# Attention, spatial gating and a feed-forward on one core: weights by output halves, VectorE turns of the late weights, four token staging tiles

## The reference, cut to what matters

```python
# attention: B=2, H=8, S=768, D=64; 8 global keys, 96 local keys, linear bias per head
scores = q @ k.T / 8 + bias; keep = is_global | is_local
x = softmax(where(keep, scores, -1e9)) @ v             # -> [2, 768, 512]
h = relu(x @ w_in)                                     # 512 -> 1024
u, v = h[..., :512], h[..., 512:]
v_n = (v - mean(v)) / sqrt(var(v) + 1e-6)              # over the 512 columns
x = (u * (w_spatial @ v_n + b_spatial[:, None])) @ w_out   # w_spatial 768 x 768
u = x + (x.T @ U @ V).T                                # rank 32 over the sequence
out = u + relu(u @ w_ch1) @ w_ch2                      # 512 -> 2048 -> 512
```

## Time and profile before

| | us |
|---|---|
| median of 3 runs | 559.49 |
| the three runs | 559.15, 559.49, 563.11 |
| profiled execution | 562.82 |
| its span | 560.7 |
| PE busy | 533.7 (95%) |
| VectorE busy | 289.5 (52%) |
| ScalarE busy | 174.3 (31%) |
| GpSimd busy | 112.0 (20%) |
| mean granted clock of TensorE | 0.98 of full speed |

### The profile page before, as it was taken

One profiled execution on the slowest core, in us unless ns is written; L12 is line 12 of the kernel. 1 busy time (PEld: TensorE's weight loads), 2 busy tenths in 40 slices (PEclk: granted clock), 3 DMA queues, 4 the chain that ended last, 5 costly groups with the idle time before them and its releaser, 6 DMA issues.

```text
span 560.7 us, 7652 instructions
## 1 busy us (share of the span) xinstructions
PE 533.7 (95%) x2728; PEld 418.3 (75%) x2728; DVE 289.5 (52%) x845; ACT 174.3 (31%) x429; POOL 112.0 (20%) x134
## 2 busy tenths in 40 slices
PE   7688999899999999999989999999999999999996
PEld 5455666567777788878768888888888888888884
DVE  5748888857775534689822265523146524011012
ACT  4755665645555533332311101021010102101010
POOL 5884000000000001498389500000000000000000
PEclk8969999989999999999989999999999999999999
DMA  7975454545514000055223100002000002000002
GB/s 179 226 158 130 102 102 105 119 97 130 122 47 129 29 30 0 2 168 161 84 76 112 39 0 1 0 1 75 1 0 2 0 2 75 1 0 1 0 1 79
DMA packets 45835, 36.25 MB, mean 65 GB/s; under 512 B 29504, under 2 KB 39744, under 8 KB 45792
## 3 DMA queue, kind: packets, MB, share of 16 engines
q1 hardware_dynamic: 39776, 19.34, 15.6%
q0 software_dynamic: 3216, 11.63, 6.9%
q10 hardware_dynamic: 2800, 4.72, 2.9%
HBM read 32.54 MB, written 3.15 MB: 64 GB/s over the span
## 4 chain that ended last, share of the span: by engine, by line
PE 80%; DVE 10%; POOL 4%; issue 3%; DMA 2%; ACT 1%; DVEq 0%; POOLq 0%; ACTq 0%
PE ps L1255 66%; PE ps L1228 5%; PE ps L1299 4%; PE ps L1272 4%; DVE uT_first L1051 2%; DMA w_raw<-in_moe_w_in 2%; POOL win_lo L464 2%; DVE pr L923 1%; PE ps L1390 1%; POOL win_hi L462 1%; DVE uT_lo L1058 1%; DVE wspT_lo L1010 1%; DVE sc L907 1%; DVE gv_lo L991 1%; POOL small L486 0%
## 5 line engine op out<-in xcount | busy, mean ns | idle before, releaser
L1176 DVE SCALAR_TENSOR_TENSOR hT_lo<-ps,hT_hi 128x512 fp32r<-128x512 f32 x48 | 33.2, 692 | 171.4 <-ACT hT_hi L773 171.4
L773 ACT ACTIVATE hT_hi<-ps 128x512 fp32r<-128x512 f32 x48 | 28.8, 599 | 228.2 <-PE ps L1255 228.2
L597 ACT ACTIVATE pr<-sc,small 128x256 f32<-128x256 f32 (+1 forms) x96 | 46.2, 483 | 52.2 <-DVE small L907 46.8
L907 DVE CUSTOM_DVE_ANT_0 sc<-ps,bias 128x256 f32<-128x256 f32 (+1 forms) x96 | 35.0, 400 | 22.8 <-PE ps L1272 21.2
L1255 PE MATMUL ps<-win_hi,xT_hi 128*128 128x512 f32 x96 | 40.9, 427 | 0.0
L1051 DVE STREAM_TRANSPOSE ys<-tokens 32x128 f32<-32x128 f32 x128 | 38.7, 302 | 1.8
L1255 PE MATMUL ps<-uT_hi,w1a_hi 128*128 128x512 f32 x96 | 38.0, 396 | 1.0 <-DVE uT_lo L1058 1.0
L1255 PE MATMUL ps<-win_hi,xT_lo 128*128 128x512 f32 x96 | 38.5, 401 | 0.0
L1255 PE MATMUL ps<-win_lo,xT_hi 128*128 128x512 f32 x96 | 38.4, 400 | 0.0
L1255 PE MATMUL ps<-uT_lo,w1a_hi 128*128 128x512 f32 x96 | 38.1, 397 | 0.0
L1255 PE MATMUL ps<-uT_hi,w1a_lo 128*128 128x512 f32 x96 | 38.0, 396 | 0.0
(11 more groups left out here) (154 smaller groups left out, 1096.4 us busy)
## 6 DMA issues: line engine op xcount, KB each, us to landing
w_raw<-in_moe_w_ch POOLq DMA_DIRECT2D x16, 512.0 KB, 4.0
wsp<-in_moe_w_spatial ACTq DMA_DIRECT2D x12, 384.0 KB, 3.7
vn<-in_v SPq DMA_DIRECT2D x12, 256.0 KB, 3.7
out<-ys SPq DMA_DIRECT2D x12, 256.0 KB, 2.2
qk_late<-in_q SPq DMA_DIRECT2D x24, 112.0 KB, 3.5
qk_late<-in_k SPq DMA_DIRECT2D x24, 112.0 KB, 3.7
vp<-in_v SPq DMA_DIRECT2D x10, 224.0 KB, 4.5
w_raw<-in_moe_w_in POOLq DMA_DIRECT2D x4, 512.0 KB, 6.0
```

Source lines behind the costliest of these rows:

```text
L597: act.activation(pr[:, k % 3, e, 0:w], sc[:, k % 2, e, 0:w], ACT.Exp, bias=nmax[:, k % 2, e:e + 1], scale=-1.0, accum_out=sums[:, k % 3, e ...
L773: act.activation(hT[0][:, n % 2, :], h1_ps(n), ACT.Relu).then_inc(s["hT_hi"], 1)
L907: dve.tensor_tensor_reduce(out=sc[:, k % 2, e, 0:w], in0=scores_ps(k, e)[:, 0:w], in1=bias[:, 2 * p + e, WINDOW - w:WINDOW], scale=-SCALE, ...
L1176: dve.scalar_tensor_tensor(hT[1][:, n % 2, :], h1_ps(n), 0.0, hT[0][:, n % 2, :], ALU.max, ALU.subtract).then_inc(s["hT_lo"], 1)
```

## The change

- **W_in by output halves.** A chunk is now two row blocks x 512 columns: V's columns of rows 0 to 255, of rows 256 to 511, then U's. Each U/V piece waits for as many chunks as it needs. LAG is 6, so pieces ride in units 6 to 29, and the product stage takes one more unit.
- **U and V** of the low-rank step are loaded with tile 4 by SP, and split later, V in four pieces after the scales of tiles 4 and 5. The scales of tiles 0 to 2 stand between the weight chunks.
- **Normalisation.** Statistics one unit later, `normed` and `gv_lo` in the first and second unit after; ACT's `gv_hi` at the start of a unit.
- **x buffers** alternate up to tile 7 (PAIRED) instead of tile 5.
- **Spatial weights of batch 1** are loaded as blocks by ACT (four DMAs a tile instead of one), turned by DVE (`turn_wsp`) into SBUF, and split from there; odd tiles have buffers of their own. PE's 12 groups of three transposes for batch 1 go.
- **Last tiles of U/V of batch 1**: V of tile 5 comes before U of tile 4.
- **First four token tiles.** DVE turns a tile in one instruction (`turn_rows`) into a staging tile `u_rows`, as soon as its tokens are done, during U/V of batch 1; SP moves the 32x32 blocks to their place with 16 DMAs a tile. ACT's `uT_hi` comes a step earlier and waits for all 64. The first `hidden` of the feed-forward comes before the low rank of tile 4 and the projection of tile 5.

```diff
-LAG = 7
+LAG = 6
+PAIRED = (ALONE + NP) // NP
+        u_rows = sb("u_rows", [P, TB, CM, TURNS, TURN])
...
-            return ps[:, 6 + (tile % 2 if tile < NT else 0), :]
+            return ps[:, 6 + (tile % 2 if tile < PAIRED else 0), :]
...
-                return w_in[c * P:(c + 1) * P, :], [w[:, c, :] for w in win]
+                at, n = c % 2 * 2, slice((1 - c // 2) * DM, (2 - c // 2) * DM)
+                return (w_in[at * P:(at + 2) * P, n].rearrange("(a p) n -> p a n", p=P),
+                        [w[:, at:at + 2, n] for w in win])
...
+            for n in range(TB):
+                sp.wait_ge(s["u_blocks"], n + 1)
+                for x in range(TURNS):
+                    for y in range(TURNS):
+                        sp.dma_start(uT_first[y * TURN:(y + 1) * TURN, :, n * P + x * TURN:n * P + (x + 1) * TURN],
+                                     u_rows[x * TURN:(x + 1) * TURN, n, :, y, :]).then_inc(s["u_moved"], 16)
...
-            split_u_v()
-            for m in range(NT):
+                if n >= ready["in"] - 1:
+                    deviation(n - ready["in"] + 1)
+            split_u((0, 1))
+            deviation(3)
+            split_u((3,))
+            split_u_low()
+            for m in (4, 5):
+                if m > 4:
+                    pool.wait_ge(s["v4_split"], 2 * (m - 4))
                 deviation(m)
+                pool.wait_ge(s["rstd_ready"], m + 1)
+                for n in (0, 1):
+                    split_v(2 * (m - 4) + n)
...
+            def load_blocks(t):
+                if t < NT:
+                    for y in range(TURNS):
+                        act.dma_start(wsp_blocks(t)[y * TURN:(y + 1) * TURN, :, :, :].rearrange("p a k c -> p (a k) c"),
+                                      blocks_d[t, y, :, :, :]).then_inc(s[f"blocks_loaded{t % 2}"], 16)
...
-                act.wait_ge(s["u_turned"], tb * TB + j + 1)
+                if tb == 0:
+                    act.wait_ge(s["u_moved"], 16 * TURNS * TURNS * TB)
...
-                    if b and 0 < t <= TB:
-                        uT_hi(0, t - 1)
+                    if b and t < TB:
+                        uT_hi(0, t)
...
+            def turn_wsp(t):
+
+                dve.wait_ge(s[f"blocks_loaded{t % 2}"], 16 * TURNS * (t // 2 + 1))
...
+                for h in range(2):
+                    half = slice(h * HALF, (h + 1) * HALF)
+                    dve.transpose(wsp_turned[t % 2][:, half, :].rearrange("p k (r a) -> p a k r", a=TURNS),
+                                  wsp_blocks(t)[:, :, half, :]).then_inc(s["wsp_turned"], 1)
...
+            def turn_rows(n):
+
+                wait(dve, "u_ready", n + 1)
+                dve.transpose(u_rows[:, n, :, :, :].rearrange("p c y r -> p (c y) r"),
+                              tokens[:, n, :].rearrange("p (m r) -> p m r", r=TURN)).then_inc(s["u_blocks"], 1)
...
+            def u_v_late(b, t, wide):
+                for q in (0, 1):
+                    u_v_piece(b, t, q, wide)
+                for q in (2, 3):
+                    if t == NT - 1:
+                        u_v_piece(b, t - 1, q, wide)
+                for q in (2, 3):
+                    if t != NT - 2:
+                        u_v_piece(b, t, q, wide)
...
-                    if (t, q) == (0, 0):
-                        pe.wait_ge(s["chunk_split"], ready["in"])
-                    if t >= 0 and q == 0:
-                        wait(pe, "xT_lo", t + 1)
...
-                wait(pe, "wspT_lo", 2 * B * NT)
+                hidden(0)
                 low_rank(1, NT - 2, True)
-                hidden(0)
                 project(1, NT - 1, True)
```

More of the change, by code:

```diff
@@ L314, in program @@
             xT_hi xT_lo uv v_done u_relu v_relu stats_ready meanvar_ready var_ready rstd_ready normed
-            gv_hi gv_split wsp_transposed wspT_hi wspT_lo mixed gate gate_transposed gT_hi gT_lo
+            gv_hi gv_split wsp_transposed wsp_turned wspT_hi wspT_lo mixed gate gate_transposed gT_hi gT_lo
             x2_sum x2_hi x2_split low_rank mix_hi mix_split h_ps u_ready
-            u_turned uT_hi uT_lo h1_ps hT_hi hT_lo h2 y_done y_ready""".split()}
+            u_blocks u_moved u_turned uT_hi uT_lo h1_ps hT_hi hT_lo h2 y_done y_ready""".split()}
         def wait(e, name, n):
@@ L767, in window @@
                     relus(1, t, True)
-                gv_hi(1, NT - 1)
+                    if t <= 2:
+                        for h in range(2):
+                            wsp_hi(1, t - 1, h, True)
+                        load_blocks(t + 1)
             def hT_hi(n):
@@ L1063, in products @@
                     gate(b, t, True)
[L1064 to L1065 removed]
+                    if b and t + 2 < NT:
+                        turn_wsp(t + 2)
+                    if b == 0 and t + 1 < NT:
+                        for h in range(2):
                             wsp_lo(b, t + 1, h, True)
[L1067 to L1069 removed]
+                    if b and 0 < t <= TB:
+                        uT_lo(0, t - 1)
                     if t:
@@ L1072, in products @@
                     gT_lo(b, t)
-                    for x in range(2, TURNS):
-                        if b and t < TB:
-                            turn_tokens(t, x)
-                    if b and t >= 2:
-                        uT_lo(0, t - 2)
+                    for h in range(2):
+                        if b and t + 2 < NT:
+                            wsp_lo(b, t + 2, h, True)
             def every():
@@ L1101, in every @@
                         apart(dve)
-                    for h in range(2):
-                        wsp_lo(b, 0, h, True)
+                    for t in range(b + 1):
+                        if b:
+                            turn_wsp(t)
+                        for h in range(2):
+                            wsp_lo(b, t, h, True)
                     for t in range(NT):
                         layer_norm(b, t)
+                        if b and t < TB:
+                            turn_rows(t)
                     gv_lo(b, NT - 1)
@@ L1171, in window @@
                     layer_norm(1, t)
+                    if 2 <= t:
+                        turn_rows(t - 2)
+                    if 2 <= t <= 3:
+                        for h in range(2):
+                            wsp_lo(1, t - 2, h, True)
                 gv_lo(1, NT - 1)
@@ L1293, in probs_v @@
                     pe.wait_ge(s[f"v_loaded{buf}"], 16 * values_loaded(tile))
-                    wait(pe, "xT_lo", tile if tile > NT else tile - 1)
+                    wait(pe, "xT_lo", tile if tile > PAIRED else tile - 1)
                 values = [vp, vn] if tile % NT else [vn]
```

211 lines of the change are left out of this document (143 added, 68 removed).

## The result

| | before | after |
|---|---|---|
| median, us (4 runs each) | 559.89 | 565.76 |
| profiled execution | 562.82 | 563.56 |
| its span | 560.7 | 561.7 |

The ratio is 1.0095, 95% interval 1.0049 to 1.0141: about 1% slower, against 552.0 forecast and outside the range of 542 to 560. The two profiled executions differ by 1.0 us of span, the medians by 5.9, because before's profiled run lay 2.9 over its median and after's 2.2 under. What follows sums the two profiles; the medians carry the verdict.

The account below looks back on a forecast made before the run. PE's work, its waits and a lowered clock were taken as the bound; 3.7 + 1.8 + 3.7 + 0.6 - 2.4 = 7.4 us off the median 559.5 gave 552.0 us, range 542 to 560.

Parts of the forecast that it names:

- Start, 3.7: Attention units 6 to 8: projection pieces a unit sooner remove the W_in wait; gain 3.7 us, bounds 0.2 and 5.4.
- Pieces of V 1.8: Near 45 us: splitting V in four pieces removes PE's wait for `pr`; gain 1.8 us, bounds 0 and 2.0.
- x buffer 3.7: Near 111 us: alternating through tile 7 removes the `xT_lo` wait and low clock; gain 3.7 us, bounds 0 and 4.6.
- I take the same difference off the median: Gains summed on the profiled execution, 3.3 us over the median, were subtracted unchanged from the median 559.49.
- A pair of transposes out of the product stage, 0.6: Product stage: VectorE turning batch 1's weights spares PE a pair of transpose groups there; gain 0.6 us.
- The last stage, -2.4: Before the feed-forward: 8.9 us go, 11.3 come from 64 SP moves at 0.46 us each; 2.4 us lost.
- rival 2: Last stage: SP's moves take longer still; at 0.75 us per DMA 18.6 us more, 570.7 us; chance 0.10.
- break-even of 0.58: Last stage: at 0.58 us per SP DMA, all other gains are eaten.
- What goes: waits of 0.9 (`gv_lo`): Last stage: PE's 0.9 us wait for `gv_lo` goes, part of the 8.9 us expected to go.
- Weight turns on VectorE, cost 0: Batch 1: first four turns fit VectorE's waits, SBUF subtractions hide behind a 4.1 us mix; 0, or 1 us lost.
- Rival 1: Last stage: the 64 DMAs keep pace with the turns and are hidden; 17.2 us gained, 542.3 us; chance 0.15.
- Rival 3: First half: start gains only 0.2 and x buffer 2.0 as clock and waits persist; 557.3 us; chance 0.20.

Follow-up runs that it names:

- e8: e4b with ACT's block loads of the spatial weights moved behind its urgent work; 548.83 us, ratio 0.981 to before.
- e12: The kernel before with only turn_rows and 16 merged moves, asked for one step later; no first half, no VectorE weight turns; 559.65 us, ratio 1.000.
- e2: The kernel before with only the staging put in: turn_rows, 64 moves by SP, ScalarE's split a step earlier; 579.47 us, ratio 1.035.
- e6: The change without VectorE's weight turns of batch 1 (PE transposes again) and without the staging (small turns again); 551.11 us, ratio 0.983 to before.
- e4b: The change with 16 merged moves instead of 64, and the moved tokens asked for one step later; 550.02 us, ratio 0.983 to before.
- e1: The change with only the staging of the first four token tiles undone (VectorE's small turns, no SP moves); 564.17 us, ratio 1.009 to before.
- e9: The change with only VectorE's weight turns of batch 1 undone (PE transposes), 64 moves asked for early; 566.83 us, ratio 1.013 to before.
- e7: e4b with VectorE's weight turns of batch 1 undone, so PE transposes the spatial weights; 544.84 us, ratio 0.973 to before.

## Why the prediction was wrong, point by point

- **Start, 3.7: the mechanism right, the size a matter of the execution.** The first piece came at 29.14 (29.2 forecast). From the head of unit 6 to that of unit 8 after took 35.13 - 28.76 = 6.37 us with one piece more than before's 10.49, so the gain is 10.49 - 6.37 + 1.36 = 5.5, the upper bound, since the clock did not fall. The wait for the scores had shrunk from 3.0 to 1.5 us, but that does not explain it. e8 has the same start and the same wait, and there the clock was 0.50 from 29 to 32, as the forecast had it. These are the two starts, after and then e8:

```profile
27.57 0.70 PE L1403 MATMUL ps<-k_turned,q_turned 64*128 64x256 f32 x4 [1.50 <-DVE small L1002]
28.76 0.63 PE L1359 MATMUL ps<-ident,pr 128*128 128x128 f32 x4 [0.49 <-issue]
```

```profile
27.58 0.70 PE L1403 MATMUL ps<-k_turned,q_turned 64*128 64x256 f32 x4 [1.50 <-DVE small L1001]
28.78 1.09 PE L1359 MATMUL ps<-ident,pr 128*128 128x128 f32 x4 [0.49 <-issue]
```

In e8 the two units took 7.94 us, a gain of 3.9. The old start varies as well: these units took 8.1 us in e12, where before's took 10.49.
- **Pieces of V 1.8, x buffer 3.7: the waits went, the sizes hung on one execution.** No wait for `pr` near 45, none for `xT_lo` near 111, full clock over 110 to 120. But e2 and e12 have before's first half, and the 2.0 us for `pr` were 0.4 and 0.95 there. Behind the same 1.96 us for `xT_lo` the clock fell in before and e2, and not in e12. Up to the first mix 13.3 us are gained on before's profile, of which one bare unit (1.85) only moved: 11.5 for 9.2 forecast. Against e12 it is 9.5, and 7.7 without that unit.
- **"I take the same difference off the median": not so.** Of the 13.8 us between 552.0 and 565.8, 8.2 lie between the profiled executions, 3.3 are this difference, and by 2.2 after's profiled execution lay under its median. The 3.3 us that before's profiled execution took beyond its median were partly the very waits and low clock that were added up as gains. The first half alone (e6) is 11.4 us shorter by the spans of its profile and before's, and 8.8 by the medians. This widened the miss; what turned a gain into a loss is the last stage, below.
- **A pair of transposes out of the product stage, 0.6: eaten.** The stage grew by 3.4 where the moved unit less this pair gives 1.25. 1.9 of the difference are the waits behind ACT's four block issues (in e8, which moved them, the stage is 1.8 us shorter than in e4b). I had counted such issues in batch 1's steps, but not the four that step 4 of batch 0's products now carries.
- **The last stage, -2.4: the step that failed.** It is the sentence "An SP issue of the same 32-row form takes 432 ns, 0.46 with the gap". The row's moves have 32 rows too, but they read from device memory. From SBUF an issue took 601 ns, and 42.4 / 64 = 0.66 with the gap. So SP ended at 255.3 instead of 252.8 - 10.0 = 242.8, and the low rank of tile 0 began at 262.1 instead of 260.2 - 10.0 = 250.2. PE came there at 262.14 - 17.23 = 244.9 instead of 252.6 - 10.0 = 242.6. 7.6 + 11.9 - 2.3 = 17.2, which is the wait measured. With 0.66 for 0.46 the forecast's own sum gives 552.0 + 64 x 0.20 = 564.8. That is rival 2, below its 0.75. The forecast's own break-even of 0.58 was passed, and its own mark for being wrong, over 36 us for the 64 issues, was met. I had bounded the issue from 0.33 to 0.75 and given the upper side 0.10 while noting that no row had SBUF as the source: the one property without a row was the one that counted.
- **"What goes: waits of 0.9 (`gv_lo`)": wrong.** It stayed; `gv_lo` still took 2.10 us beside GpSimd.
- **Weight turns on VectorE, cost 0: wrong, and hidden in this result.** They were credited with 3.5 us of PE's transposes. With the moves out of the way they cost 5 to 13. The cover I named (a mix of 4.1 us) does not hold, since VectorE runs its list in order and the gate of the next step stands behind them. The Trainium skill (SBUF — State Buffer, Who interferes with whom) spoke against this part, and I priced it at 0 or 1 us. The runs bear the page out: a pair of subtractions from SBUF took 2.68 and 3.22 us beside GpSimd's splits in e1, and 1.02 us between them.
- **Rival 1 and its page.** The Trainium skill (DMA: Bandwidth & Descriptors, Issuing engines are not separate DMA queues) calls the time to initiate a DMA usually small relative to the DMA itself. Here one issue took 0.60 us, 0.66 with the gap, against 2.3 us to landing, and the 64 in a row took 42.4 us with only the last landing behind them. The measurement decides.
- **Rival 3** did not come: the start gained more than forecast.

What stays open: how e1's 13.1 us divide between the SBUF operands, ACT's block loads and the falls of the clock beyond the 3.8 of the bare turns; and what makes the first half vary. The first mix of the old one began at 119.4, 117.5 and 115.6 in before, e2 and e12, with low clock from unit 6 on for 13.7, 6.8 and 3.4 us, and that of the new one between 104.6 and 107.7 wherever it was kept whole. What decides whether the clock falls behind a wait of 1.5 to 2 us is open too.

## What to carry to other kernels

Price a DMA issue by a row with the same source and target, not only the same shape, and where many small ones stand in front of a wait, count their issues first: fewer and larger ones (16 for 64) gained 10.8 us here without moving a byte less. An instruction that waits for a slow chain belongs behind the urgent work of its engine's list, and so do DMA issues on an engine that also computes. Undo parts one by one, in pairs too: the wait for the moves covered a second loss of the same size, and taking out the staging alone (e1) or the weight turns alone (e9) made no faster kernel than before, taking out both (e6) gave 551, and a mended staging on top (e7) 545. And compare a profiled execution with the median before its waits are added up as gains: the waits and low clock that it had beyond others are no part of a median run.

## What the runs showed of the hardware that was not expected

- SP's issue of a DMA of 32 rows took 602 and 591 ns with the source in SBUF, 432 and 422 from device memory, whether a row's 128 values were one run or four. 16 moves of four times the size took 750 ns each (median) and landed after 5.2 us instead of 2.3.
- Four DMA issues on ACT kept ACT from its next instruction for 2.3 and 2.7 us in after.
- Two subtractions of 128x384 with both operands in SBUF took 1.02 us together in e1 where GpSimd ran no split, as much as from PSUM, and 2.68 and 3.22 us beside one.
- Behind the same wait of 1.50 us the clock fell to 0.50 for some 3 us in e8 and stayed at 1.00 in after.
- A turn of 128x512 whose output elements lie side by side took 0.70 us (`turn_rows`), where one of the same size with its output elements four apart took 1.09; the weight turns, of 128x384 and also four apart, took 0.8.
